# Both matrix products of a fused dynamic convolution and feed-forward kernel read their moving operand's 512 columns from the last to the first

## The chip, the cores and the metric

The kernel runs on one core of one Trainium2 chip. The metric is the device time of one execution in microseconds (us). A core has a TensorE (PE, with its weight loads listed apart as PEld), a VectorE (DVE), a ScalarE (ACT), a GpSimd (POOL) and a SyncE (SP, which here issues all transfers), and they are ordered among each other by semaphores alone.

## The reference

```
w = softmax(weight_gen, axis=-1)            # (4, 4096, 8 heads, 7 taps)
conv[b, s, h, :] = sum_k w[b, s, h, k] * x_pad[b, s + k, h, :]   # 6 zero rows ahead, 24 channels a head
h = conv.reshape(16384, 192) @ w_in         # (192, 2048)
g = h * (1 / (1 + exp(-1.702 * h)))
out = g @ w_out                             # (2048, 192), result (16384, 192)
```

## The kernel before

The 16384 tokens are cut into 18 pieces: four narrow ones and 14 wide ones. For each piece DVE makes the convolution (lines 280 to 322), turns it with a transpose (L339) so that channels lie on partitions and tokens in columns, and the result is kept in `xt` as two float32r terms, a rounded one (ACT, L216) and its remainder (DVE, L345). A wide piece has 1024 tokens, 512 in partitions 0 to 63 and 512 in partitions 64 to 127; a narrow one has half as many, and the `cross` copies fill each half of the partitions with the other half's tokens.

The products go by units. A unit is 128 rows of the hidden layer for both halves of a piece's tokens; there are 8 units in a narrow piece and 16 in a wide one, 256 in all. Each matmul uses 64 rows of the array: `rows` is the lower or the upper half of the partitions, so two matmuls in a row (h = 0 and 1) work on different halves of the array, and they are called a pair here. Their moving operand is always 64 partitions by 512 columns of float32r, their stationary operand 64 by 128.

- `first_product` (L420, matmul on L441) makes one unit of `hid` in PSUM: three combinations of rounded and remainder terms by three slices of 32 channels, so 9 pairs. The moving operand is `xt[rows, j % 2, part, k, :]`.
- ACT applies the activation to a finished unit twice (L252 to `gate`, L255 rounded to `gate_hi`), and DVE takes the remainder (L406, `gate_lo`). All three read and write the columns in ascending order.
- `second_product` (L447, matmul in `halves`, L459) adds a unit into `acc_main` (output channels 0 to 127, 6 pairs) and `acc_rest` (channels 128 to 191, 4 pairs) in PSUM. The moving operand is `gate_hi` or `gate_lo`, as `g[rows, s, h, :]`.

So a unit has 19 pairs, and the kernel has 256 x 19 = 4864 pairs, or 9728 matmuls. TensorE's order is written out by hand: `first_product` of a unit, then `second_product` of the unit two before it (LAG = 2). The last two second products stand alone at the end. `hid` has two buffers, `gate_hi` and `gate_lo` have four slots. When a piece is through, ACT and DVE move its `acc_main` and `acc_rest` out (`lift`, L238, and `evict`, L378), and SP stores them.

In the profile a column of `64*128 64x512` in a matmul's row is the array part that it uses and its moving operand.

Of the kernel before, what the change touches and what calls it, by code (L numbers as in the profile page):

```python
# [31 lines left out]
def ffn_of_dynamic_conv(nc: bass.Bass, x_runs: bass.AP, tap_runs: bass.AP, w1_rows: bass.AP, w2_rows: bass.AP,  # L32
# [27 lines left out]
    with ExitStack() as ctx:  # L60
        def sb(name, shape, dt=F32):
            return ctx.enter_context(nc.sbuf_tensor(name, shape, dt))
# [8 lines left out]
        w2 = sb("w2", [P, CH, 2 * D], F32R)  # L71
# [13 lines left out]
        xt = sb("xt", [P, 2, 2, SLICES, N], F32R)  # L85
# [7 lines left out]
        hid = ctx.enter_context(nc.psum_tensor("hid", [P, 2, 2, N], F32))  # L93
# [25 lines left out]
        def wait(eng, s, value):  # L119
            if value > 0:  # L120
                eng.wait_ge(s, value)
# [3 lines left out]
        def is_narrow(j):  # L125
            return PIECES[j] == NARROW
# [290 lines left out]

        @block.tensor
        def _(pe):
            def first_product(j, v):  # L420
                n = UNIT0[j] + v
                q, cc = v // (CH // 2), v % (CH // 2)
                if n == UNIT0[len(NARROWS)] + CH // 2:
                    pe.wait_ge(w1_doubled, 64)
                wait(pe, gate_hi_ready, n - 1)
                f = slice(cc * P, (cc + 1) * P)
                terms = [(w, part, k) for w, part in ((w1_hi, 0), (w1_lo, 0), (w1_hi, 1)) for k in range(SLICES)]
                for i, (w, part, k) in enumerate(terms):
                    if v == 0 and i == 0:
                        pe.wait_ge(xt_hi_ready, j + 1)  # L430
                        if is_narrow(j):
                            pe.wait_ge(hi_crossed, 2 * (j + 1))
                    if v == 0 and i == 2 * SLICES:
                        pe.wait_ge(xt_lo_ready, j + 1)
                        if is_narrow(j):
                            pe.wait_ge(lo_crossed, 2 * (j + 1))
                    if n in (0, 2) and i == SLICES:
                        pe.wait_ge(w1_lo_ready, 1 + n // 2)
                    for h in range(2):
                        rows = slice(h * HALF, (h + 1) * HALF)  # L440
                        last = nc.tensor.matmul(hid[:, v % 2, h, :], w[rows, k, q, f], xt[rows, j % 2, part, k, :],  # L441
                                                start=(i == 0), stop=(i == len(terms) - 1))
                last.then_inc(hid_ready, 1)

            MAIN, REST_COLS, MAIN_LO = slice(0, P), slice(P, 2 * P), slice(2 * P, 3 * P)

            def second_product(j, v):  # L447
                n = UNIT0[j] + v
                s = v % SLOTS
                first, last_unit = v == 0, v == UNITS[j] - 1  # L450
                q, cc = v // (CH // 2), v % (CH // 2)
                chunk = (cc + q * (CH // 2), cc + (1 - q) * (CH // 2))

                def halves(acc, g, cols, crossed, start, stop):

                    for r in range(2):
                        h = 1 - r if crossed else r
                        rows = slice(r * HALF, (r + 1) * HALF)
                        done = nc.tensor.matmul(acc[:, h, :], w2[rows, chunk[h], cols], g[rows, s, h, :],  # L459
                                                start=start, stop=stop)  # L460
                    return done

                if n == 0:
                    pe.wait_ge(w2_lo_ready, 2)
                wait(pe, gate_lo_ready, n + 1)
                if first:
                    wait(pe, main_out_act, j)
                    wait(pe, main_out_dve, j)

                wait(pe, main_added, n)  # L470
                halves(acc_main, gate_hi, MAIN, False, first, False)
                halves(acc_main, gate_hi, MAIN_LO, False, False, False)
                halves(acc_main, gate_lo, MAIN, False, False, False).then_inc(main_straight, 1)
                if first:
                    wait(pe, rest_out, 2 * j)
                wait(pe, rest_added, n)
                halves(acc_rest, gate_hi, REST_COLS, True, first, False)
                halves(acc_rest, gate_lo, REST_COLS, True, False, False).then_inc(rest_crosswise, 1)
                wait(pe, main_straight, n + 1)
                halves(acc_main, gate_hi, MAIN, True, False, False)  # L480
                halves(acc_main, gate_hi, MAIN_LO, True, False, False)
                halves(acc_main, gate_lo, MAIN, True, False, last_unit).then_inc(main_added, 1)
                wait(pe, rest_crosswise, n + 1)
                halves(acc_rest, gate_hi, REST_COLS, False, False, False)
                halves(acc_rest, gate_lo, REST_COLS, False, False, last_unit).then_inc(rest_added, 1)

            for j in range(LAST + 1):
                for v in range(UNITS[j]):
                    first_product(j, v)
                    if v >= LAG:  # L490
                        second_product(j, v - LAG)
                    elif j > 0:
                        second_product(j - 1, v - LAG + UNITS[j - 1])
            for v in range(UNITS[LAST] - LAG, UNITS[LAST]):
                second_product(LAST, v)
# [40 lines left out]
```

## Time and profile before

| | |
|---|---|
| time, median of 3 runs | 1135.38 us (1135.04 to 1135.48) |
| the profiled execution | 1135.54 us |
| its span, first to last instruction | 1133.7 us |
| mean granted TensorE clock in it | 1.000 |
| PE busy | 1107.6 us, 98% |
| PEld busy | 916.2 us, 81% |
| DVE busy | 812.1 us, 72% |
| ACT busy | 620.6 us, 55% |
| transfers | 41.23 MB, mean 36 GB/s |

The span is the stretch that the trace covers; 1135.54 - 1133.7 = 1.8 us of the execution lie around it. Busy time of PE is the union of matmuls that overlap each other: each is listed with its whole passage through the array, so a mean of 386 ns for one doesn't say how often one starts. How often they start is read from their start times.

### The profile page before, as it was taken

How to read it: one execution, taken by the hardware profiler on the slowest of the kernel's cores; microseconds unless marked ns; L12 is line 12 of the kernel's file. 1: busy time of each engine (PE TensorE's matmuls, PEld its weight loads, DVE VectorE, ACT ScalarE, POOL GpSimd, SP SyncE). 2: the span in 40 equal slices, each digit the busy share in tenths (PEclk: the TensorE clock that was granted, in tenths of full speed). 3: DMA queues.
4: the chain of work that ended last, by engine and by line, in shares of the span. 5: the costliest groups of instructions: out<-in, count | busy, mean ns of one | idle time of the engine just before them, and what ended most of it. 6: DMA issues, size and time to landing. Idle time of an engine off the chain costs nothing.

```text
span 1133.7 us, 21631 instructions
## 1 busy us (share of the span) xinstructions
PE 1107.6 (98%) x9728; PEld 916.2 (81%) x9728; DVE 812.1 (72%) x709; ACT 620.6 (55%) x653; POOL 0.2 (0%) x4
## 2 busy tenths in 40 slices
PE   2999999999999999999999999999999999999998
PEld 2888788888888888888888888888888888888886
DVE  8898978769486684957859487594866849578322
ACT  5777665464554645546464554645546455454543
POOL 0000000000000000000000000000000000000000
PEclk9999999999999999999999999999999999999999
DMA  7501010100201010010100101002010100100000
GB/s 246 183 15 52 16 40 15 40 29 1 67 1 40 29 38 30 1 39 29 39 29 1 44 25 39 29 1 67 1 39 29 38 29 1 40 28 2 28 1 29
DMA packets 8348, 41.23 MB, mean 36 GB/s; under 512 B 1024, under 2 KB 1152, under 8 KB 5952
## 3 DMA queue, kind: packets, MB, share of 16 engines
q1 hardware_dynamic: 8256, 39.85, 10.8%
q8 instruction: 77, 1.26, 0.5%
q14 instruction: 15, 0.12, 0.0%
HBM read 24.12 MB, written 12.58 MB: 32 GB/s over the span
## 4 chain that ended last, share of the span: by engine, by line
PE 95%; DVE 3%; ACT 1%; issue 1%; DMA 0%; ACTq 0%; DVEq 0%
PE hid L441 45%; PE acc_main L459 30%; PE acc_rest L459 20%; DVE prod L314 1%; DVE conv L321 1%; ACT gate L252 0%; DVE conv L314 0%; DVE gate_lo L406 0%; DMA taps<-in_tap_runs 0%; ACT gate_hi L255 0%; ACT xt L225 0%; ACT xt L216 0%; ACT xt L220 0%; ACT L210 0%; DVE prod L339 0%
## 5 line engine op out<-in xcount | busy, mean ns | idle before, releaser
L252 ACT ACTIVATE gate<-hid 128x1024 f32<-128x1024 f32 x256 | 263.0, 1027 | 482.4 <-PE hid L441 482.2
L406 DVE TENSOR_TENSOR gate_lo<-gate,gate_hi 128x1024 fp32r<-128x1024 f32 x256 | 311.9, 1219 | 254.9 <-ACT gate_hi L255 254.1
L441 PE MATMUL hid<-xt,w_hi 64*128 64x512 f32 x3072 | 433.8, 388 | 20.7 <-ACT xt L235 20.6
L441 PEld LDWEIGHTS hid<-xt,w_hi 64*128 64x128 f32 x3072 | 289.9, 185 | 81.0 <-ACT xt L216 20.6
L459 PE MATMUL acc_main<-gate_hi,w 64*128 64x512 f32 x2048 | 316.0, 386 | 0.4 <-DVE outs_main L381 0.4
L255 ACT ACTIVATE gate_hi<-hid 128x1024 fp32r<-128x1024 f32 x256 | 261.2, 1020 | 0.0
L459 PEld LDWEIGHTS acc_main<-gate_hi,w 64*128 64x128 f32 x2048 | 192.3, 184 | 40.7 <-issue 1.1
L441 PE MATMUL hid<-xt,w_lo 64*128 64x512 f32 x1536 | 217.0, 388 | 0.0
L459 PE MATMUL acc_rest<-gate_hi,w 64*128 64x512 f32 x1024 | 200.0, 387 | 0.0
L459 PE MATMUL acc_main<-gate_lo,w 64*128 64x512 f32 x1024 | 199.8, 386 | 0.0
L459 PE MATMUL acc_rest<-gate_lo,w 64*128 64x512 f32 x1024 | 199.7, 386 | 0.0
L321 DVE TENSOR_TENSOR conv<-conv,prod 128x1536 f32<-128x1536 f32 (+1 forms) x108 | 169.8, 1573 | 0.1
L314 DVE TENSOR_TENSOR prod<-xwin,tap_norm 128x1536 f32<-128x1536 f32 (+1 forms) x108 | 168.8, 1575 | 1.3
L441 PEld LDWEIGHTS hid<-xt,w_lo 64*128 64x128 f32 x1536 | 145.5, 185 | 29.8
L459 PEld LDWEIGHTS acc_rest<-gate_hi,w 64*128 64x128 f32 x1024 | 96.2, 184 | 21.0 <-DVE outs_rest L384 1.3
L459 PEld LDWEIGHTS acc_main<-gate_lo,w 64*128 64x128 f32 x1024 | 96.3, 184 | 19.8
L459 PEld LDWEIGHTS acc_rest<-gate_lo,w 64*128 64x128 f32 x1024 | 96.3, 184 | 19.7
L381 DVE COPY outs_main<-acc_main 128x512 f32<-128x512 f32 x18 | 12.4, 689 | 44.1 <-PE acc_main L459 44.1
L216 ACT ACTIVATE xt<-prod 128x1536 fp32r<-128x1536 f32 (+1 forms) x18 | 24.3, 1348 | 12.9 <-DVE prod L339 12.9
L314 DVE TENSOR_TENSOR conv<-xwin,tap_norm 128x1536 f32<-128x1536 f32 (+1 forms) x18 | 28.4, 1579 | 1.6
L339 DVE STREAM_TRANSPOSE prod<-conv 128x1536 f32<-128x1536 f32 (+1 forms) x18 | 28.8, 1600 | 0.6
L384 DVE TENSOR_TENSOR outs_rest<-acc_rest,outs_rest 64x512 f32<-64x512 f32 x36 | 23.0, 677 | 8.6 <-ACT outs_rest L245 8.6
(28 smaller groups left out, 197.5 us busy)
## 6 DMA issues: line engine op xcount, KB each, us to landing
xwin<-in_x_runs SPq DMA_DIRECT2D x15, 1056.0 KB, 5.0
out<-outs_main SPq DMA_DIRECT2D x13, 512.0 KB, 2.7
out<-outs_rest SPq DMA_DIRECT2D x13, 256.0 KB, 2.9
taps<-in_tap_runs SPq DMA_DIRECT2D x1, 3136.0 KB, 15.5
taps<-in_w_rows SPq DMA_DIRECT2D x2, 1536.0 KB, 9.2
w_hi<-w_hi SPq DMA_DIRECT2D x2, 768.0 KB, 8.2
w_lo<-w_lo SPq DMA_DIRECT2D x2, 768.0 KB, 7.2
out<-outs_main SPq DMA_DIRECT2D x6, 256.0 KB, 2.1
```

Of the source, the lines that this page charges most:

```text
L216: nc.scalar.activation(own(j, 0), turned(j), ACT.Copy).then_inc(xt_hi_ready, 1)
L252: nc.scalar.activation(gate[:, v % 2, :, :], hid[:, v % 2, :, :], ACT.Gelu_apprx_sigmoid).then_inc(gate_ready, 1)
L255: nc.scalar.activation(gate_hi[:, v % SLOTS, :, :], hid[:, v % 2, :, :], ACT.Gelu_apprx_sigmoid).then_inc(gate_hi_ready, 1)
L314: nc.vector.tensor_tensor(to.rearrange("p (g c) -> p g c", c=GRP), xwin[:, at:at + u, :].rearrange("p t (h c) -> p (t h) c", c=GRP), norm[ ...
L321: nc.vector.tensor_tensor(acc, acc, prod[:, k % 2, 0:u * CB], ALU.add).then_inc(conv_ready if last else conv_op, 1)
L339: nc.vector.transpose(turned(j).rearrange("p k (u i) -> p u k i", i=LANES), conv[:, 0:PIECES[j] * CB].rearrange("p (u k c) -> p u k c", k= ...
L381: nc.vector.tensor_copy(outs_main[:, 1, :], acc_main[:, 1, :]).then_inc(main_out_dve, 1)
L384: nc.vector.tensor_tensor(outs_rest[:, h, :], acc_rest[0:HALF, h, :], outs_rest[:, h, :], ALU.add).then_inc(rest_out, 1)
L406: nc.vector.tensor_tensor(gate_lo[:, v % SLOTS, :, :], gate[:, v % 2, :, :], gate_hi[:, v % SLOTS, :, :], ALU.subtract).then_inc(gate_lo_r ...
L441: last = nc.tensor.matmul(hid[:, v % 2, h, :], w[rows, k, q, f], xt[rows, j % 2, part, k, :], start=(i == 0), stop=(i == len(terms) - 1))
L459: done = nc.tensor.matmul(acc[:, h, :], w2[rows, chunk[h], cols], g[rows, s, h, :], start=start, stop=stop)
```

## The change

A slice that steps by -1 over the last dimension is put in the place of the full ascending slice in the moving operand of both matmuls. Column i of `hid` then holds what column 511 - i held. The activation and the remainder keep this reversed order in `gate_hi` and `gate_lo`, and the second product reads them reversed in turn, so `acc_main` and `acc_rest` have their columns as before. The written columns of every matmul go up as before, and stationary operands, semaphores, instruction counts and transfers stay.

```diff
         @block.tensor
         def _(pe):
+
+            BACK = slice(None, None, -1)
+
             def first_product(j, v):
...
-                        last = nc.tensor.matmul(hid[:, v % 2, h, :], w[rows, k, q, f], xt[rows, j % 2, part, k, :],
+                        last = nc.tensor.matmul(hid[:, v % 2, h, :], w[rows, k, q, f], xt[rows, j % 2, part, k, BACK],
                                                 start=(i == 0), stop=(i == len(terms) - 1))
...
-                        done = nc.tensor.matmul(acc[:, h, :], w2[rows, chunk[h], cols], g[rows, s, h, :],
+                        done = nc.tensor.matmul(acc[:, h, :], w2[rows, chunk[h], cols], g[rows, s, h, BACK],
                                                 start=start, stop=stop)
```

## Rows read from the trace of the kernel before

**Rows 1.** The page: busy time, share of the span and instructions of each engine.
```profile
PE 1107.6 (98%) x9728; PEld 916.2 (81%) x9728; DVE 812.1 (72%) x709; ACT 620.6 (55%) x653; POOL 0.2 (0%) x4
```

**Rows 2.** The page, the chain that ended last: shares of the span by engine.
```profile
PE 95%; DVE 3%; ACT 1%; issue 1%; DMA 0%; ACTq 0%; DVEq 0%
```

**Rows 3.** Stretches of the span: us, busy time of each engine (instructions), granted clock, DMA share, GB/s.
```profile
0.00:20.60 20.60, 0.00 (x0) 0.00 (x0) 16.63 (x23) 10.17 (x7) 0.20 (x4) 1.00 0.92 301
180.00:1130.00 950.00, 948.71 (x8372) 783.68 (x8368) 654.33 (x526) 502.95 (x528) 0.00 (x0) 1.00 0.08 26
```

**Rows 4.** The chain by time: start us, length us, what; two units 212 apart and the end.
```profile
202.51 2.04 PE hid L441 x18
204.55 0.68 PE acc_main L459 x6
...
1115.52 2.04 PE hid L441 x18
...
1128.30 0.02 ACT outs_main L241
```

**Rows 5.** Matmuls and weight loads, 180 to 1120 us: duration ns min/median/max, starts, forms.
```profile
L441 PE MATMUL hid<-xt,w_hi x2620: 386/386/386, 180.8 to 1119.9; 64*128 64x512 f32 x188
L459 PE MATMUL acc_main<-gate_hi,w x1748: 386/386/386, 179.7 to 1118.8; 64*128 64x512 f32 x195
L441 PEld LDWEIGHTS hid<-xt,w_hi x2622: 184/184/184, 180.6 to 1119.9; 64*128 64x128 f32 x188
```

**Rows 6.** Groups, 180 to 1120 us: busy us, mean ns, idle before and what ended it.
```profile
L441 PE MATMUL hid<-xt,w_hi 64*128 64x512 f32 x2620 | 368.0, 386 | 0.0
L252 ACT ACTIVATE gate<-hid 128x1024 f32<-128x1024 f32 x219 | 225.0, 1027 | 433.4 <-PE hid L441 433.2
L406 DVE TENSOR_TENSOR gate_lo<-gate,gate_hi 128x1024 fp32r<-128x1024 f32 x219 | 267.1, 1220 | 239.1 <-ACT gate_hi L255 238.5
```

**Rows 7.** PE by time near the start of the products: start us, length us, instruction.
```profile
21.64 0.66 PE L441 MATMUL hid<-xt,w_hi 64*128 64x512 f32 x2
22.07 0.66 PE L441 MATMUL hid<-xt,w_lo 64*128 64x512 f32 x2
22.49 0.66 PE L441 MATMUL hid<-xt,w_lo 64*128 64x512 f32 x2
22.92 0.66 PE L441 MATMUL hid<-xt,w_lo 64*128 64x512 f32 x2
23.34 0.68 PE L441 MATMUL hid<-xt,w_hi 64*128 64x512 f32 x2
```

**Rows 8.** Groups of the whole span with shapes apart: two DVE operations, each at two sizes.
```profile
L321 DVE TENSOR_TENSOR conv<-conv,prod 128x1536 f32<-128x1536 f32 x84 | 147.0, 1750 | 0.0
L314 DVE TENSOR_TENSOR prod<-xwin,tap_norm 128x1536 f32<-128x1536 f32 x84 | 146.2, 1753 | 0.9
L321 DVE TENSOR_TENSOR conv<-conv,prod 128x768 f32<-128x768 f32 x24 | 22.8, 951 | 0.1
L314 DVE TENSOR_TENSOR prod<-xwin,tap_norm 128x768 f32<-128x768 f32 x24 | 22.6, 953 | 0.4
```

## The prediction

> **What bounds the kernel now.** I read the shares of busy time first: PE has 1107.6 of 1133.7 us, while DVE has 812.1 and ACT 620.6 [rows 1]. A busy share alone could hide stalls inside a matmul's listed length, so the chain that ended last comes next: 95% of it is PE [rows 2]. The stretches then show where the rest is. PE does nothing for 20.6 us at the start, and between 180 and 1130 us it is busy for 948.71 of 950 us, although its matmuls end at 1128.3 us, so it has no gaps at all there [rows 3, 4]. In that stretch no matmul group has idle time before it, while ACT sits 433.2 us waiting for PE and DVE 238.5 us waiting for ACT [rows 6]. So every engine behind PE has slack, and PE has none.
>
> What sets PE's own pace is the number that matters here, and it can't be read from the length of a matmul (386 ns, [rows 5]), because matmuls overlap. From the chain by time: one unit's first product starts at 202.51 us and another's at 1115.52 us, 212 units later [rows 4]. That is 913.01 / 212 = 4.307 us for a unit of 19 pairs, or 226.7 ns for a pair. 512 columns at the clock's upper level of 2.4 GHz are 213.3 ns, and the granted clock is 1.00 in this stretch [rows 3]. So a pair spends 213.3 ns on one column per cycle and 13.4 ns on something else. The two matmuls of a pair run side by side in different halves of the array, so 226.7 ns is the pace of one stream of 512 columns.
>
> The weight loads are 184 ns each [rows 5], and those of a pair also run side by side, so they fit under 226.7 ns with 43 ns to spare.
>
> The model for the whole: 20.6 us before the first matmul, 256 units x 4.307 = 1102.6 us, 1128.3 - 20.6 - 1102.6 = 5.1 us of slower first matmuls and small waits, 5.4 us of moving out and storing behind the last `acc_main` (to the span's end at 1133.7), 1133.7 in all, and 1.8 us around the span give the profiled execution's 1135.54 us. The median of the runs is 1135.38, 0.16 us lower; the sum is made against the profiled execution and then moved by that much.
>
> **The change, part by part.**
>
> *Instructions.* None is added or removed: 9728 matmuls and 9728 weight loads as in [rows 1]. The step is a field of the operand's address pattern. Cost 0.
>
> *Stationary operand.* Not touched. The 184 ns of a load stay and stay hidden.
>
> *Written columns.* `hid`, `acc_main` and `acc_rest` are written upwards as before. Only the data in `hid` is permuted. Cost 0 for TensorE and for those who read `hid`: L252, L255 and L406 see the same shapes and the same order of addresses (1027, about 1020 and 1220 ns; they have the slack of [rows 6] in any case).
>
> *Waits.* PE waits for whole semaphore counts before a first product (`xt_hi_ready`, `xt_lo_ready`) and before a second (`gate_lo_ready`), never for part of a tile. Which column is read first makes no wait longer. On each side the readers of a tile wait for its last column. Cost 0.
>
> *Reading 512 float32r columns downwards.* This is the one unknown, and it comes 9728 times, in 4864 pairs. No instruction of this trace reads downwards. I bound it from three rows.
> - Nearest from below: 0. The pace of 226.7 ns is 13.4 ns over the columns themselves. If the order of reading had any share in these 13.4 ns, the most that a better order could give back is 13.4 x 4864 = 65 us. I see no reason for any of it: both orders touch the same 2048 bytes of each partition once, in one unbroken run.
> - Nearest pattern that isn't a plain ascending run: on DVE, L314 multiplies by a tap that is read again and again (a step of 0 over 24 channels), where L321 adds two plain runs. 1753 against 1750 ns at 1536 elements, 953 against 951 at 768 [rows 8]: the unusual pattern costs 2 to 3 ns an instruction and nothing per element. On PE that would be 2 to 3 ns x 4864 pairs = 9.7 to 14.6 us, if it can't be hidden by the neighbour half.
> - Farthest: the reading gets slower per column. The only slower pace of the same instruction that the trace shows is at the start: pairs start at 21.64, 22.07, 22.49, 22.92 and 23.34 us [rows 7], so 1.70 / 4 = 425 ns a pair, which is 512 columns at 1.2 GHz, the clock's lower level (the granted clock is given as 1.00 there too, but the pace says otherwise; PE had done nothing for 20.6 us before). A stream fed at half speed would look like this: (425 - 226.7) x about 4850 pairs = 962 us more.
>
> I take 0: address patterns that aren't plain ascending runs cost 0.2 to 0.3% on the engine where the trace has both kinds, and a step of -1 leaves four neighbouring elements next to each other in time, as a step of 1 does.
>
> A page speaks to this. The Trainium skill ("Advanced Engine Details and Errata", section Memory Cachelines) says that SBUF is read in lines of 16 bytes, that at least two accesses in a row to one line are needed to hide the memory's latency, and that an operand that changes line at each access pays. By that rule a downward run of four-byte elements still touches each line four times in a row and has the same 128 line changes as an upward one, so the sum stays at 1135.4 us. No row here shows a line or its cost. The same section says of PSUM that a non-contiguous pattern slows matmuls down a lot; the pattern on the PSUM side isn't changed, and whether hardware counts a downward run as contiguous the section doesn't say.
>
> Sum: 1135.54 + 0 = 1135.5 us for a profiled execution, and 1135.4 us beside a median of 1135.38.
>
> **The rivals.**
>
> *A. No difference* (the forecast): 1135.4 us. For it: same bytes, same number of columns, nothing else on the path.
>
> *B. Slower: TensorE's reader is fed at full pace only by an ascending run.* Where it fetches more than one column at a time and keeps what it fetched only for the next higher column, each column downwards needs a fetch of its own. It decides as soon as such a fetch takes longer than one column at 2.4 GHz (0.42 ns), because PE has no slack at all; at half speed a pair takes 425 ns, and the time is 1135.4 + 962 = 2097 us. For it: every moving operand in this kernel is ascending and contiguous, so the trace never tries anything else, and 4 bytes a partition per 0.42 ns is the fastest stream of any engine here (DVE's 1753 ns for 1536 elements is 1.14 ns an element). Against it: two engines' patterns cost next to nothing in [rows 8], though neither steps downwards. Should the fetch be only a little short, the time would be anywhere between. The Trainium skill's rule on lines would exclude this case; its rule on PSUM, if it were applied to a downward run on the SBUF side, would be this case.
>
> *C. Slightly slower: a fixed charge per matmul*, for instance for the start at the far end of a row. At 2 to 3 ns a pair: 1145 to 1150 us.
>
> *D. Faster: part of the 13.4 ns belongs to the ascending order*, for instance because both halves' reads or the rows that ACT and DVE write upwards at the same time meet the reads less often. All of it would be 65 us, 1070 us; a tenth would be 6.5 us, 1129 us. Against it: PE's matmuls are 386/386/386 ns (shortest, median, longest) over a stretch in which ACT and DVE are now busy and now idle [rows 3, 5]. If writes beside the reads cost anything, these lengths would spread.
>
> *E. The change doesn't do what it says*: the pattern is turned back to an ascending one on its way to the chip. The output would still be right, since each product would be unreversed. The time is A's, and only an edit that makes the order visible in the output would tell them apart.
>
> **How the numbers follow.** A with E has 0.78, B 0.12, C 0.07, D 0.03. The range has to leave out no more than 2 in 10. B lies far off, at up to 2097 us, and leaving it out costs 0.12, so the range is A with the small charge of C: from 1132 us (the spread of the runs and a small part of D) to 1150 us (3 ns a pair). It holds 0.78 + 0.07 = 0.85 by my cases. A measurement of this kernel can tell about 0.2%, 2.3 us, from no change; A and E lie within it, C and B are slower, D is faster: faster 0.03, same 0.78, slower 0.19.
>
> **What would show it.** If A holds, the matmuls of the middle stretch are 386 ns again, loads 184 ns, a unit 4.307 us, ACT waits about 433 us for PE there. In B the unit's length grows (8.1 us at half speed), weight loads stay short or wait for their turn, and ACT's and DVE's waits for PE grow by the same sum; the cold pairs at the start tell what kind of limit it is: they stay at 425 ns if the reader has a pace of its own, and grow if it needs more cycles of PE's clock. In C only some ns are added to each pair, and the two products show them alike. The forecast is wrong if the start-to-start time of pairs moves by more than 0.45 ns, since that alone is 2.2 us over 4864 pairs.

## The result

The changed kernel takes 1164.93 us (median, 1164.36 to 1165.4) where the kernel before took 1135.43 us: 29.5 us more, a ratio of 1.026 (95% interval 1.0243 to 1.0278). The forecast was 1135.4 us, no change, with a range of 1132 to 1150. The measured time lies 15 us above the range.

The page of the changed kernel, its busy times and its chain's shares (they answer to [rows 1] and [rows 2]):

```profile
PE 1137.1 (98%) x9728; PEld 917.0 (79%) x9728; DVE 812.0 (70%) x709; ACT 621.5 (53%) x653; POOL 0.2 (0%) x4
PE 98%; DVE 1%; ACT 0%; DMA 0%; issue 0%; ACTq 0%; DVEq 0%
```

PE is 29.5 us longer with the same 9728 matmuls; weight loads, DVE and ACT are where they were. So nothing else became the bound: the matmuls themselves are slower. The matmuls and weight loads between 180 and 1120 us, with duration in ns (shortest, median, longest), as in [rows 5] (lines 441 and 459 are 444 and 462 now):

```profile
L444 PE MATMUL hid<-xt,w_hi x2544: 394/394/394, 181.8 to 1119.1; 64*128 64x512 f32 x196
L462 PE MATMUL acc_main<-gate_hi,w x1698: 394/394/394, 179.7 to 1119.6; 64*128 64x512 f32 x189
L444 PEld LDWEIGHTS hid<-xt,w_hi x2544: 185/185/185, 181.6 to 1118.9; 64*128 64x128 f32 x196
```

A matmul is listed with 394 ns instead of 386, the shortest as the longest, and in both products alike. What counts is how often they start. The chain by time, start and length in us, at the two units that [rows 4] shows, in the changed kernel:

```profile
204.18 2.10 PE hid L444 x18
206.28 0.70 PE acc_main L462 x6
...
1144.04 2.10 PE hid L444 x17
```

These are the same two units, 212 apart, as the ones at 202.51 and 1115.52 us before. (1144.04 - 204.18) / 212 = 4.433 us a unit instead of 4.307, which over 19 pairs is 233.3 ns instead of 226.7. Between these two points the changed kernel loses 28.52 - 1.67 = 26.85 us, and 212 x 19 x 6.67 ns are 26.87. 6.67 ns is 16 cycles at 2.4 GHz.

All 4864 pairs at 6.67 ns would be 32.4 us, but the span grew by 28.9 (1162.6 - 1133.7). The missing 3.5 us lie ahead of the unit at 202.51, where the changed kernel is only 1.67 us late and 41 units x 0.127 = 5.2 us would be due. Two things take it back. The first is the start. The first 54 matmuls in the chain, changed kernel, then before, then an experiment below that also reads its lines upwards:

```profile
20.50 8.23 PE hid L444 x54
```
```profile
20.65 9.28 PE hid L441 x54
```
```profile
20.66 8.56 PE hid L445 x54
```

TensorE starts at the lower of its two clock levels: pairs start 427 ns apart, until 23.65 us in the changed kernel and until 26.78 us before, and at the upper level's pace after that. Two kernels that both read upwards differ by 0.7 us in these 54 matmuls (9.28 and 8.56 us), so this varies without a change of the reading order, and the 3.1 us between before and changed are not put down to the change. The earlier rise of the clock and the earlier first matmul put the changed kernel 1.2 us ahead at the 55th matmul (28.57 against 29.76 us), where it should be 0.2 us behind. The second is small waits, of which the slower kernel has hardly any. PE in the stretch from 120 to 140 us (length, busy time, clock, share of transfers), before, then changed:

```profile
120.00:140.00 20.00, 19.62 (x170) 1.00 0.07 21
```
```profile
120.00:140.00 20.00, 20.00 (x174) 1.00 0.07 21
```

In the narrow pieces of the beginning DVE has more to do than later (before, it is busy for 121.97 of 140 us from 40 to 180 us, and for 654.33 of 950 us after that), and the chain of the kernel before runs over it from 118 to 132 us. By the start times of the matmuls, pairs that start late add up to 2.3 us before and to 0.2 us in the changed kernel, between the 55th matmul and the unit at 202.51. This gives 2.1 us back: 5.2 - 1.4 - 2.1 = 1.7. From there to the unit at 1115.52 us every unit has the same length, in either kernel.

### The profile page after: what moved, and what is told of

Same layout as the page of the kernel before. It is cut to its first block, busy times and chain, and to the rows that moved or that the text cites. A ratio compares the mean times of both kernels' runs of the same rounds, so it can differ in the third digit from the quotient of the medians.

```text
span 1162.6 us, 21631 instructions
## 1 busy us (share of the span) xinstructions
PE 1137.1 (98%) x9728; PEld 917.0 (79%) x9728; DVE 812.0 (70%) x709; ACT 621.5 (53%) x653; POOL 0.2 (0%) x4
## 4 chain that ended last, share of the span: by engine, by line
PE 98%; DVE 1%; ACT 0%; DMA 0%; issue 0%; ACTq 0%; DVEq 0%
PE hid L444 46%; PE acc_main L462 31%; PE acc_rest L462 21%; DVE prod L314 0%; DVE conv L321 0%; DMA taps<-in_tap_runs 0%; DVE prod L339 0%; DVE conv L314 0%; ACT xt L235 0%; ACT xt L216 0%; ACTq L60 0%; DVE outs_rest L384 0%; DVEq L60 0%; DVE tap_norm L298 0%; DVE taps L333 0%
## 5 line engine op out<-in xcount | busy, mean ns | idle before, releaser
L252 ACT ACTIVATE gate<-hid 128x1024 f32<-128x1024 f32 x256 | 263.1, 1028 | 513.0 <-PE hid L444 512.8
L406 DVE TENSOR_TENSOR gate_lo<-gate,gate_hi 128x1024 fp32r<-128x1024 f32 x256 | 311.8, 1219 | 281.7 <-ACT gate_hi L255 280.9
L444 PE MATMUL hid<-xt,w_hi 64*128 64x512 f32 x3072 | 443.3, 395 | 20.5 <-ACT xt L235 20.5
L462 PE MATMUL acc_main<-gate_hi,w 64*128 64x512 f32 x2048 | 322.9, 394 | 0.0
L255 ACT ACTIVATE gate_hi<-hid 128x1024 fp32r<-128x1024 f32 x256 | 261.4, 1021 | 0.0
L444 PE MATMUL hid<-xt,w_lo 64*128 64x512 f32 x1536 | 221.8, 395 | 0.0
L462 PE MATMUL acc_rest<-gate_hi,w 64*128 64x512 f32 x1024 | 203.6, 394 | 0.0
L462 PE MATMUL acc_main<-gate_lo,w 64*128 64x512 f32 x1024 | 203.4, 394 | 0.0
L462 PE MATMUL acc_rest<-gate_lo,w 64*128 64x512 f32 x1024 | 203.4, 394 | 0.0
L314 DVE TENSOR_TENSOR prod<-xwin,tap_norm 128x1536 f32<-128x1536 f32 (+1 forms) x108 | 168.9, 1576 | 1.3
L314 DVE TENSOR_TENSOR conv<-xwin,tap_norm 128x1536 f32<-128x1536 f32 (+1 forms) x18 | 28.4, 1580 | 1.6
```

The source lines that it names most:

```text
L252: nc.scalar.activation(gate[:, v % 2, :, :], hid[:, v % 2, :, :], ACT.Gelu_apprx_sigmoid).then_inc(gate_ready, 1)
L255: nc.scalar.activation(gate_hi[:, v % SLOTS, :, :], hid[:, v % 2, :, :], ACT.Gelu_apprx_sigmoid).then_inc(gate_hi_ready, 1)
L314: nc.vector.tensor_tensor(to.rearrange("p (g c) -> p g c", c=GRP), xwin[:, at:at + u, :].rearrange("p t (h c) -> p (t h) c", c=GRP), norm[ ...
L406: nc.vector.tensor_tensor(gate_lo[:, v % SLOTS, :, :], gate[:, v % 2, :, :], gate_hi[:, v % SLOTS, :, :], ALU.subtract).then_inc(gate_lo_r ...
```

## Experiments

Each edit is against the changed kernel. Paces are the mean distance of two pairs, from the start times of the units between 310 and 900 us in the trace; for before it is 226.7 ns and for the changed kernel 233.3. Most kernels ran twice, and the times of one kernel agree within 0.3% except where it is said.

**One half of the array alone reads downwards.**

```diff
-    ... xt[rows, j % 2, part, k, BACK]
+    ... xt[rows, j % 2, part, k, slice(None) if h else BACK]
-    ... g[rows, s, h, BACK]
+    ... g[rows, s, h, slice(None) if h else BACK]
```

> In both products the matmul of the pair that works on h = 0 reads its 512 columns last to first, the one on h = 1 first to last. The output is whole. In the changed kernel all 4864 pairs start 233.3 ns apart (2.10 us for 9), before 226.7 (2.04 us for 9), so 6.67 ns more. Theory 1, each half of the array has its own reader and a downward stream costs a fixed 6.67 ns more in it: the slower half sets the pace, pairs 233.3 ns apart, median about 1165 us. Theory 2, the charge grows with the columns read, each half with its own reader: the same, 233.3 ns and 1165 us. Theory 3, both matmuls of a pair go one after another through one shared stage and each downward one pays 3.33 ns there: pairs 230.0 ns apart, median about 1150 us.

1161.33 us, 1.0235 of before (1.0218 to 1.0252); 232.6 ns. Its chain around 301 us:

```profile
301.23 2.10 PE hid L444 x18
303.33 0.70 PE acc_main L462 x6
304.03 0.47 PE acc_rest L462 x4
304.50 0.68 PE acc_main L462 x6
305.18 0.47 PE acc_rest L462 x4
305.65 2.10 PE hid L444 x18
```

Theory 3 (one shared stage, 230.0 ns) falls. Theories 1 and 2 gave 233.3, and the trace shows where the 0.7 ns less come from. The first product's matmuls are of two kinds here:

```profile
L444 PE MATMUL hid<-xt,w_lo x1056: 386/390/394, 182.3 to 956.4; 64*128 64x512 f32 x176
```

In one unit, of every second matmul four start at 460.072, 460.299, 460.526, 460.752 us, 226.7 ns apart and each listed with 386 ns. Of the ones between, four start at 460.419, 460.652, 460.886, 461.119 us, 233.3 ns apart and each listed with 394 ns. So each half of the array has a stream of its own and keeps its own pace, and the upward half runs ahead: the downward one is 116 ns behind it at the unit's start and 199 ns behind after 13 pairs. Then the halves change roles (`crossed` in `halves`), and once in a unit the half that is ahead waits (one distance of 298 ns). The half that reads downwards in 14 of a unit's 19 pairs needs 14 x 233.3 + 5 x 226.7 = 4400 ns, and that explains most of the 4.420 us a unit instead of 4.433. The other 20 ns are not explained.

**Fewer columns, upwards and downwards.** With M = 448 and then 480:

```diff
+                m = N if n < 2 else M
...
-    nc.tensor.matmul(hid[:, v % 2, h, :], ..., xt[rows, j % 2, part, k, BACK],
+    nc.tensor.matmul(hid[:, v % 2, h, 0:m], ..., xt[rows, j % 2, part, k, slice(m - 1, None, -1)],
```

(`slice(0, m)` upwards; the second product likewise, with all columns in unit 0 alone. These kernels leave a part of the output out.)

> Ascending, but only the first 448 of the 512 columns are multiplied in both products (all 512 in the first unit or two, so that PSUM holds defined values); the last 64 columns of each half piece are left out. 64 columns are 26.7 ns at 2.4 GHz. If the 13.4 ns that a pair takes over its columns are fixed: 200.0 ns a pair, about 1135.4 - 26.67 x 4860 / 1000 = 1006 us. If they grow with the columns: 198.3 ns a pair, about 998 us. If the weight loads (184 ns) or another engine take over, more than 200 ns.

> As the ascending kernel of 448 columns, with the same 64 columns of each half piece left out, but the 448 are read last to first. Theory 1 (fixed charge for a stream): 6.67 ns a pair more than the ascending 448-column kernel, 206.7 ns where that has 200.0. Theory 2 (charge grows with the columns): 6.67 x 448 / 512 = 5.83 ns more, 205.8 ns. If descending reads were a matter of slack beside the weight loads, the difference would be near 0. In time about 30 us (theory 1) or 26 us (theory 2) over the ascending one.

1041.06 us and 204.8 ns upwards, 1051.72 us and 207.1 ns downwards. The difference is 2.3 ns, neither theory's number, and the pairs are no longer evenly spaced in either kernel, with the weight loads of 184 ns close behind. So fewer columns were taken away:

> Ascending, with 480 of 512 columns multiplied (all 512 in the first unit or two); the last 32 columns of each half piece are left out. 448 columns came close to the weight loads of 184 ns, and their pairs were no longer evenly spaced, so this takes fewer away. If the 13.3 ns over the columns are fixed: 200.0 + 13.3 = 213.3 ns a pair, about 1135 - 13.33 x 4860 / 1000 = 1070 us. If they grow with the columns: 212.5 ns, 1066 us.

> As the ascending kernel of 480 columns, with the same 32 columns left out, read last to first (479 to 0). Theory 1 (a fixed charge for a stream): 6.67 ns more than that kernel's pairs, 220.0 ns where it has 213.3. Theory 2 (the charge grows with the columns or lines): 6.67 x 480 / 512 = 6.25 ns more, 219.6 ns.

1091.85 us and 216.7 ns upwards, 1105.46 us and 220.0 ns downwards. Take the columns' own time off (186.7 ns at 448, 200.0 at 480, 213.3 at 512, all at 2.4 GHz). Downwards 20.4, 20.0 and 20.0 ns are left: nearly a fixed amount for a stream. But upwards it is 18.2, 16.7 and 13.3 ns. So the difference between the two orders is not fixed: 2.3, 3.3 and 6.67 ns at 448, 480 and 512 columns, where theory 1 had 6.67 at 480 and theory 2 had 6.25. The upward stream is the one whose overhead varies, which no theory had foreseen.

**Runs of 256 columns downwards, the runs upwards.**

```diff
+            def in_runs(columns):
+                return columns.rearrange("p (b i) -> p b i", i=256)
...
-    nc.tensor.matmul(hid[:, v % 2, h, :], ..., xt[rows, j % 2, part, k, BACK],
+    nc.tensor.matmul(in_runs(hid[:, v % 2, h, :]), ..., in_runs(xt[rows, j % 2, part, k, :])[:, :, ::-1],
```

(the second product likewise; the next experiments change the run's length `i` and the index only.)

> Both products read two runs of 256 columns, each last to first, the lower run first (columns 255 to 0, then 511 to 256). The output is whole, since the second product undoes the first one's order. Theory 1 (fixed charge for a stream, whatever its length or order): 233.3 ns a pair, about 1165 us. Theory 1b (fixed charge for each downward run that begins): 6.67 more for the second run, 240.0 ns, about 1194 us. Theory 2 (charge by columns read downwards): 233.3 ns, 1165 us. If only a pattern with a step of -1 in a single dimension is slow: less than 233.3.

1164.76 us and 233.3 ns: theory 1b (a charge for each downward run) falls.

**Runs of 4 columns, one 16-byte line each: turned inside (`i=4`, `[:, :, ::-1]`), and then in downward order with each line read upwards (`i=4`, `[:, ::-1, :]`).**

> Both products read 128 runs of 4 columns (16 bytes), each run last to first, the runs in ascending order: 3, 2, 1, 0, 7, 6, 5, 4 and on. The output is whole. Theory E (each step of -1 or each element read against the order costs, or the innermost step's sign does): 233.3 ns a pair, 1165 us. Theory L (what costs is that the 16-byte lines come in descending order): 226.7 ns, 1135 us. If each begun downward run costs something: far more, 128 x 6.67 ns = 850 ns a pair at the worst.

> Both products read 128 runs of 4 columns (16 bytes), each run first to last, the runs in descending order: 508 to 511, 504 to 507 and on. The output is whole. Theory L (lines in descending order cost): 233.3 ns a pair, 1165 us. Theory E (the innermost step's sign costs): 226.7 ns, 1135 us. If a jump to another line breaks a read ahead: far more than 233.3.

1134.94 us for the first (ratio to before 1.0001, 0.999 to 1.0013), 1164.41 us for the second (1.0259). The first product's matmuls between 180 and 1120 us, of the first kernel (226.7 ns a pair) and then of the second (233.3):

```profile
L445 PE MATMUL hid<-xt,w_hi x2622: 386/386/386, 179.9 to 1119.2; 64*128 64x512 f32 x188
```
```profile
L445 PE MATMUL hid<-xt,w_hi x2544: 394/394/394, 181.8 to 1119.1; 64*128 64x512 f32 x196
```

This pair separates best. 384 of 511 steps go down in the first kernel, and it costs nothing; 384 of 511 steps go up in the second, and it costs all of it. Theory E (the sign of the step) falls and theory L stands: the order of the 16-byte lines matters, and the order of the four columns in one does not. Nor does a pattern of two dimensions cost anything by itself. One rival wasn't tried: every kernel here writes its columns upwards in PSUM, so the runs don't tell a downward reading from a reading against the written order.

**Two halves of a row in exchanged order (`i=256`, `[:, ::-1, :]`).**

> Both products read the columns 256 to 511 first to last and then 0 to 255 first to last, so one step of the whole stream goes down and it starts in the middle. The output is whole. Theory S (a stream costs more when it starts above its lowest line or ends below its highest): 233.3 ns a pair, 1165 us. Theory L (each descending step from line to line takes its share of the 6.67 ns): 1 of 127 steps, 226.7 ns, 1135 us.

1134.67 us and 226.7 ns (ratio 0.9999, 0.9988 to 1.001). A stream may start in the middle and jump back once at no cost: theory S falls.

**Runs of 8 and of 16 columns turned inside (`i=8` and `i=16`, `[:, :, ::-1]`).**

> Both products read 64 runs of 8 columns (32 bytes, 2 lines), each run last to first, the runs ascending. The output is whole. Runs of 16 cost 40.0 ns a pair for 31 upward jumps between runs. If each jump of more than one line costs 1.25 to 1.3 ns: 63 jumps, about 80 ns more, 307 ns a pair and 1520 us. If a block of 32 bytes is read as one: 226.7 ns, 1135 us. If 64-byte blocks read downwards are what costs: 226.7 to 233.3 ns.

> Both products read 32 runs of 16 columns (64 bytes, 4 lines of 16 bytes), each run last to first, the runs ascending. The output is whole. Theory L (16-byte lines are the unit, and 96 of 127 steps between lines go down): 5.0 ns more a pair if it goes by steps (231.7 ns, 1158 us), 6.67 if it is there or not (233.3, 1165). Theory B (the unit is a block of 64 bytes or more, and its inside is free): 226.7 ns, 1135 us.

(The kernel with runs of 16 came first.) Runs of 8 give 1164.53 us and 233.3 ns: to exchange every two neighbouring lines already costs the full 6.67 ns. That is the upper end of the third guess, and neither the 80 ns nor the nothing of the other two. Runs of 16 give 1326.89 us, 1.169 of before, and 266.7 ns. The chain of that kernel, two units:

```profile
301.41 2.40 PE hid L445 x18
...
306.48 2.40 PE hid L445 x18
```

5.07 us a unit, 40 ns more a pair than before. None of the theories gave that. So the charge doesn't grow with the number of downward steps between lines (all 127: 6.67 ns; 64, in runs of 8: 6.67; 96, in runs of 16: 40), and what makes 64-byte runs so bad stays open.

**The tiles moved by 4 bytes.** `xt`, `gate_hi` and `gate_lo` become slices of tiles that are 64 bytes longer, and begin SHIFT elements in. So `xt` moves by the shift alone, `gate_hi` by 64 bytes more and `gate_lo` by 128 more; the expectations name the shift only.

```diff
+        def shifted(name, shape, letters):
...
+            whole = sb(name, [P, count + 16], F32R)
...
+            return whole[:, SHIFT:SHIFT + count].rearrange(...)
-        xt = sb("xt", [P, 2, 2, SLICES, N], F32R)
+        xt = shifted("xt", [2, 2, SLICES, N], "abcd")
```

> All reads ascending as before the change, but the tiles xt, gate_hi and gate_lo begin one element (4 bytes) later, so every row of 512 columns begins at 4 bytes past a multiple of 64 and ends in the next such block. The output is whole. Theory A (place: a stream costs more by how its first or last word lies in aligned blocks of 16 or 64 bytes, and a downward stream merely starts at the end of one): up to 233.3 ns a pair, 1165 us. Theory D (direction: any downward stream costs 6.67 ns more, wherever it lies): 226.7 ns a pair, as before, 1135 us.

> All reads last to first as in the changed kernel, with xt, gate_hi and gate_lo one element later, so that each downward stream starts in the first word of an aligned block of 16 and of 64 bytes instead of the last. The output is whole. Theory A (place of the start in its block): something other than 233.3 ns, 226.7 if the start in the last word was what cost, 240 if it is the number of blocks touched. Theory D (direction alone): 233.3 ns a pair and 1165 us.

1183.67 us and 236.1 ns upwards, 1176.93 us and 235.8 ns downwards. The two runs upwards lie 0.8% apart (1179.12 and 1188.23 us), and the pace is that of the faster one. In it a row that begins inside a line costs 9.5 ns a pair upwards, more than the change under study, and downwards 2.5 on top of the 6.67. Place matters, so theory D (direction alone) is not the whole, but the start in the last word of a line isn't what the changed kernel pays for either, since a start in a first word gave nothing back.

**By whole lines: 16 bytes in both directions, 64 bytes upwards.** As above with SHIFT = 4 and 16.

> All reads last to first, with xt, gate_hi and gate_lo 16 bytes (one line of 4 columns) later, weights where they were. The output is whole. Theory W: the moving reads stand one line further against the weight reads, so a pair takes something other than 233.3 ns. Theory D: 233.3 ns and 1165 us.

> All reads first to last as before the change, with xt, gate_hi and gate_lo 16 bytes (one line) later. The output is whole. Theory D, and if a shift by 4 bytes cost only because streams then begin inside a line: 226.7 ns, 1135 us. Theory W: the relative place changes, so something other than 226.7 ns is possible (236 at a shift of 4 bytes).

> All reads first to last, with xt, gate_hi and gate_lo 64 bytes (four lines, 16 columns) later. The output is whole. If the place within a 64-byte block decides: 226.7 ns a pair and 1135 us, as without a shift. If any change of place against the weights or against a larger block takes the favourable pace away: about 231 ns and 1155 us, as at a shift of one line.

Downwards 1164.45 us and 233.3 ns: no difference. Upwards 1155.13 us and 231.2 ns at 16 bytes, 1155.4 us and 231.2 ns at 64, each 1.018 of before (1.0149 to 1.0209 at the widest). A unit's first product, whose moving operand `xt` moved by exactly the shift, in the chains of the kernel at 16 bytes and of the one at 64:

```profile
299.91 2.08 PE hid L454 x18
304.30 2.07 PE hid L454 x18
```
```profile
300.45 2.07 PE hid L454 x18
304.83 2.07 PE hid L454 x18
```

Before it was 2.04 [rows 4], and 2.10 downwards. So the place in a 64-byte block isn't it: an upward stream at another place, lines aligned, costs 4.6 of the 6.67 ns as well. At 16 bytes the start times show more than the mean does: the distance of two pairs runs from 225 to 235 ns, and each of a unit's 19 pairs has the same distance, within 1 ns, in all units between 220 and 1100 us. So it depends on which pair of the unit it is, and each pair has its own weights and its own slice of the moving tile. The shifts move the rows that ACT and DVE write as well, and this wasn't tested apart.

**Weight loads that read one line.**

```diff
+            def one_column(weights):
+                return weights[:, 0:1].broadcast_to(weights.shape)
-    ... w[rows, k, q, f], ...          ... w2[rows, chunk[h], cols], ...
+    ... one_column(w[rows, k, q, f])   ... one_column(w2[rows, chunk[h], cols])
```

> As the changed kernel (moving operand last to first), but every weight load reads one column of its 128 over and over (a step of 0), so it touches a single line instead of 32; the products then have the wrong weights, which is the part that is changed. Theory W (the 6.67 ns come from the moving reads meeting the weight load's reads): 226.7 ns a pair or less, about 1135 us. Theory D (a descending stream pays by itself): 233.3 ns, 1165 us.

> As the kernel before (moving operand first to last), with every weight load reading one column of its 128 over and over, so the products have the wrong weights. Control for the kernel above: theory D 226.7 ns a pair, 1135 us; theory W 226.7 ns, or less (down to 215) if even the 13.3 ns over the columns come from such meetings.

Downwards 1164.84 us and 233.3 ns, upwards 1156.15 us and 231.1 ns (1.0188 of before, 1.0159 to 1.0218). Matmuls of the first product from 180 to 1120 us, upwards with such loads:

```profile
L447 PE MATMUL hid<-xt,w_hi x2568: 385/392/393, 181.7 to 1118.9; 64*128 64x512 f32 x198
```

The downward stream doesn't gain from it, so theory W, as it was meant (the 6.67 ns are meetings of the two readers), falls. But the upward stream loses 4.4 ns by a change of the weight loads alone, and its matmuls are no longer equally long (385 to 393 ns). So how the weights are read does have a share in how fast an upward stream runs.

The paces together, ns a pair at 512 columns:

| moving operand | as placed | 16 bytes on | 64 bytes on | 4 bytes on | one-line weights |
|---|---|---|---|---|---|
| lines upwards | 226.7 | 231.2 | 231.2 | 236.1 | 231.1 |
| lines downwards | 233.3 | 233.3 | not run | 235.8 | 233.3 |

## Why the prediction was wrong

*What bounds the kernel:* right. PE was the bound and is (98% of the chain), no new wait arose, and every ns of a pair's pace counted 4864 times but for the 3.5 us that the start took back. The pace of 226.7 ns as columns plus 13.4 ns was the right thing to work out.

*The parts at zero* (instructions, weight loads, written columns, waits): right. Same counts, loads of 185 ns hidden under 233.3, no wait in PE's way; ACT's and DVE's groups took the same times (1028, 1021 and 1219 ns; before 1027, 1020 and 1220). Only that a hidden load costs nothing was too simple a picture: with one-line loads, hidden as well, an upward pair takes 4.4 ns more.

*The price of a downward read:* this is the step that failed. It was put at 0, with a bound of 2 to 3 ns a pair from the DVE rows [rows 8], and it is 6.67 ns a pair. Two faults, the first of them argued and not shown: DVE takes 1.14 ns for an element and TensorE 0.42, so an irregularity that DVE hides may stand open on TensorE. And a step of 0 isn't a step of -1, nor does L314 take its lines downwards. The row was the nearest in the trace, but it was not near. (Its 3 of 1750 and 2 of 951 ns are also 0.2%, not "0.2 to 0.3%".) The argument that each line is touched four times in a row was checked only for what happens inside a line.

*Rival B* (a fetch for each column downwards) named a stream that TensorE feeds less well downwards, and put it at up to 962 us. The mechanism is refuted: order inside a line is free (1134.94 us). Its milder form, a reader that is fed a little short when the lines don't come upwards, is closer to what the runs show than its price was. *Rival C* (a fixed charge for each matmul), given 0.07, came nearest: every pair pays the same here, and what a downward stream has over its columns is 20.0 ns at 480 and at 512 alike. It was mis-sized, 6.67 ns against 2 to 3, so 1145 to 1150 us stood where 1164.9 came, and the range ended below it. And the far end of a row isn't what is paid for: with the two halves exchanged the reading starts in the middle and costs nothing, and against an upward stream of 480 columns the charge is only 3.3 ns. *Rival D* said that part of the 13.4 ns could belong to the ascending order's place: there is such a dependence, but the kernel before already stands on its favourable side, and it is the change and the shifts that leave it. *Rival E* falls with the result: the same work in another order took another time.

*What would show it:* the pace moved by more than 0.45 ns, as the text had asked for. The cold pairs at the start stayed: in the changed kernel one starts at 22.77 us, the next at 23.20.

```profile
22.77 0.66 PE L444 MATMUL hid<-xt,w_lo 64*128 64x512 f32 x2
23.20 1.13 PE L444 MATMUL hid<-xt,w_hi 64*128 64x512 f32 x6
```

At the lower clock level 512 columns take 426.7 ns and neither the 13.3 nor the 20.0 ns are to be seen: pairs start 427 ns apart in both kernels, and so they do even in the kernel of 16-column runs, at 21.481, 21.908 and 22.335 us, which takes 266.7 ns at the upper level. Whatever the extra time is, it is hidden behind the columns there. By the test that the prediction set, this speaks for a limit with a pace of its own and not one in TensorE's cycles. But a plain pace for each column would have given 218.8 ns at 480 columns downwards (233.3 x 480 / 512), and it was 220.0, so what kind of limit it is stays open.

*The Trainium skill's rule* ("Advanced Engine Details and Errata", Memory Cachelines) that lines are 16 bytes and that accesses in a row to one line run at full pace agrees with the kernel of 4-column runs turned inside: 226.7 ns with lines upwards and columns turned. What the rule leaves out decided here, that a changed order of the lines has a price: 233.3 ns with lines downwards, though each line is still read four times in a row. The measurement decides, and reading four columns of a line in a row is not enough.

What stays open is the mechanism behind it. Shown: the charge belongs to each half's stream, it comes with lines out of upward order (though a single jump back costs nothing), a downward stream has 20.0 ns over its columns at 480 and at 512, and neither a place 16 bytes on nor one-line weight loads take that away. Not shown: what in the reader it is, why an upward stream has 13.3 ns over its columns at this place and 17.9 at others, and why 64-byte runs turned inside cost 40. Weights read in the other direction and columns written downwards were not tried. Nor was a place found that is better than the kernel's own.

## What to carry to other kernels

Where TensorE is the bound and its stream has no slack, as here, the order of a moving operand is not free: keep its 16-byte lines ascending and its rows starting on a line, and put a reversal, if one is needed, inside lines or where another engine has time (the last is advice, no run here tried it). A tile's place is worth a try too: 16 bytes on cost 4.6 ns a pair here. A pattern's price read from one engine doesn't bound its price on a faster one, so give an operation that the trace never shows a wide range, above all when it is repeated thousands of times on the path: 3 ns here are 15 us. And look for what the slower engine gives back: 2.1 us of the loss were covered by waits that only the faster kernel had to sit through.

## What the runs showed of the hardware that was not expected

- A reversed moving operand of 512 float32r columns, against the upward one at the same place, costs 6.67 ns a stream, 16 cycles at 2.4 GHz, and the columns inside a 16-byte line may be read in either order at no cost (226.7 ns).
- The two halves of the array read at their own paces at the same time: 226.7 ns upwards beside 233.3 ns downwards.
- An upward stream is sensitive to where it lies: 13.3 ns over its columns as placed, 17.9 when moved by 16 or 64 bytes, 22.8 when moved by 4. A downward one has 20.0 as placed and 16 bytes on, and 22.5 when moved by 4.
- Runs of 64 bytes turned inside cost 40 ns a stream (1326.89 us), six times what a fully reversed operand costs.
- Weight loads that read a single column 128 times take 184 to 185 ns like any other, and slow an upward moving stream by 4.4 ns.
